# Layer two of a gated scan with two Strassen-like MLPs: who takes the finished sums out of PSUM

## The reference, cut to what matters

```python
# x, f_logit: (1, 6080, 256); lower_bound: (256); d_ff = 2048, fp32 throughout
f = lower_bound + (1 - lower_bound) * sigmoid(f_logit)
h[t] = f[t] * h[t-1] + (1 - f[t]) * x[t]            # a scan over 6080 tokens
# layer one: 6080 x 256 -> 2048 -> 256
a = h @ moe_w_in;  g = maximum(0.01 * a, a);  y = g @ moe_w_out
# layer two: the same shapes
a = y @ moe2_w_in
g = where(a >= 1, a, where(a <= -1, 0, (a + 1) ** 2 / 4))
out = g @ moe2_w_out                                # (6080, 256), row-major in HBM
```

## Time and profile before

| | |
|---|---|
| median of 3 runs | 1038.54 us |
| the profiled execution's own time | 1038.13 us |
| its span, first to last instruction | 1036.3 us |
| mean granted TensorE clock | 0.994 of full |
| TensorE matmul busy | 1004.5 us, 97% |
| VectorE busy | 802.8 us, 77% |
| ScalarE busy | 678.1 us, 65% |
| GpSimd busy | 197.5 us, 19% |

### The profile page before, as it was taken

How to read it: one execution, slowest core, us unless ns; L and a number is a source line. 1 busy time by engine, 2 the same in 40 slices (tenths; PEclk the granted TensorE clock), 3 DMA queues, 4 the chain that set the end, 5 groups by cost and what they waited for, 6 DMA issues and landing times.

```text
span 1036.3 us, 11820 instructions
## 1 busy us (share of the span) xinstructions
PE 1004.5 (97%) x4387; PEld 820.2 (79%) x4387; DVE 802.8 (77%) x823; ACT 678.1 (65%) x955; POOL 197.5 (19%) x191
## 2 busy tenths in 40 slices
PE   7999999999999999999989989999999999999996
PEld 6888788888888888888868868877877786887885
DVE  4766678678667677654688898898889889888885
ACT  5776777767767777756656665665666666666653
POOL 3404144333323300040040050040004005000000
PEclk8999999999999999999999999999999999999999
DMA  7433323334344230154330012011110201100112
GB/s 197 103 79 71 70 89 87 122 79 105 117 108 116 97 62 1 43 198 156 112 101 1 1 41 36 6 40 21 21 41 1 41 1 38 25 17 1 21 21 38
DMA packets 160605, 65.45 MB, mean 63 GB/s; under 512 B 142754, under 2 KB 150052, under 8 KB 160548
## 3 DMA queue, kind: packets, MB, share of 16 engines
q1 hardware_dynamic: 152516, 48.02, 19.5%
q0 software_dynamic: 3584, 15.73, 4.1%
q10 hardware_dynamic: 4448, 0.95, 0.5%
HBM read 40.70 MB, written 23.99 MB: 62 GB/s over the span
## 4 chain that ended last, share of the span: by engine, by line
PE 77%; DVE 12%; ACT 5%; issue 3%; DMA 1%; SPq 1%; POOL 0%; DVEq 0%; ACTq 0%
PE S L1074 39%; PE U L1058 34%; DVE G L863 3%; PE U L1025 3%; DVE H L858 2%; DVE H L838 2%; ACT G L592 2%; DVE extra L853 2%; ACT keep L557 2%; DVE H L846 1%; ACT extra L572 1%; DVE VF L820 1%; SPq L285 1%; DVE extra L878 1%; DMA extra<-in_f_logit_dram 1%
## 5 line engine op out<-in xcount | busy, mean ns | idle before, releaser
L1074 PE MATMUL S<-G,W_down 128*128 128x512 f32 (+2 forms) x2304 | 568.4, 388 | 3.3 <-DVE G L863 3.3
L1074 PEld LDWEIGHTS S<-G,W_down 128*128 128x128 f32 x2304 | 432.8, 188 | 92.4 <-DVE G L863 3.1
L1058 PE MATMUL U<-VF,W_up 128*128 128x512 f32 (+1 forms) x1848 | 467.1, 392 | 16.8 <-DVE H L846 10.0
L1058 PEld LDWEIGHTS U<-VF,W_up 128*128 128x128 f32 x1848 | 342.9, 188 | 103.4 <-ACT keep L557 14.1
L557 ACT ACTIVATE keep<-U 128x512 f32<-128x512 f32 (+1 forms) x352 | 207.6, 590 | 185.1 <-PE U L1058 184.8
L863 DVE TENSOR_TENSOR G<-H,G 128x1024 fp32r<-128x1024 f32 (+3 forms) x208 | 249.1, 1198 | 101.9 <-ACT G L592 100.7
L592 ACT ACTIVATE G<-H 128x1024 fp32r<-128x1024 f32 (+3 forms) x208 | 200.8, 985 | 7.4 <-DVE H L858 5.0
L572 ACT ACTIVATE extra<-extra,half 128x1024 f32<-128x1024 f32 (+1 forms) x96 | 109.3, 1140 | 118.2 <-DVE extra L853 117.9
L858 DVE SCALAR_TENSOR_TENSOR H<-H,extra 128x1024 f32<-128x1024 f32 (+1 forms) x96 | 123.1, 1291 | 34.5 <-ACT extra L572 34.5
L846 DVE TENSOR_TENSOR H<-U,keep 128x1024 f32<-128x1024 f32 (+1 forms) x88 | 107.2, 1218 | 44.9 <-ACT keep L557 43.8
L838 DVE TENSOR_TENSOR H<-U,keep 128x1024 f32<-128x1024 f32 (+1 forms) x88 | 106.7, 1213 | 29.4 <-PE U L1058 19.5
(11 more groups left out here) (76 smaller groups left out, 345.0 us busy)
## 6 DMA issues: line engine op xcount, KB each, us to landing
ready_up<-G POOLq DMA_DIRECT2D x8, 896.0 KB, 3.9
W_up<-ready_up SPq DMA_DIRECT2D x8, 896.0 KB, 5.0
extra<-in_f_logit_dram SPq DMA_DIRECT2D x44, 128.0 KB, 3.3
extra<-in_x_dram SPq DMA_DIRECT2D x44, 128.0 KB, 3.4
middle<-sent SPq DMA_DIRECT2D x22, 256.0 KB, 2.7
V<-middle SPq DMA_DIRECT2D x5, 1024.0 KB, 5.1
out_dram<-extra SPq DMA_DIRECT2D x40, 128.0 KB, 2.7
ready_down<-G POOLq DMA_DIRECT2D x8, 512.0 KB, 2.9
```

What stands on the lines that cost most here:

```text
L1058: mm = nc.tensor.matmul(U[:, bank, 0:w], w_form(j, wp, a), v_form(stage, vp, b), start=fresh and i == 0, stop=i == 2, skip_group_check=True)
L1074: mm = nc.tensor.matmul(S[:, 2 * d + h, 0:w], W_down[:, j, wp, at], g_of(u, e, gp)[:, h * w:(h + 1) * w], start=j == 0 and e == 0 and k == ...
```

## The change

For the stages of layer two but the last, `turn` now reads the finished bank in PSUM (`S`) instead of ScalarE's copy in `sent`, and ScalarE's four `take` calls in unit j = 1 are gone. The four turns of a stage move from the ends of units j = 2 and 3 into unit j = 1 of the next stage: two ahead of `add_second_chunk`, two behind it. TensorE, before it writes a bank anew, waits for the turn of that bank (`s_turned`) where it waited for the take (`s_taken`). Layer one, the first stage of layer two (which follows layer one's last tile) and the final turns are as they were. It concerns five places: the starts of the stages two to six of layer two.

```diff
 # ScalarE, unit loop of layer two
-                if u > SECOND + 1 and j == 1 and live:
-                    take(s - 1, 0)
-                    take(s - 1, 1)
...
-                if u > SECOND + 1 and j == 1 and live:
-                    take(s - 1, 2)
-                    take(s - 1, 3)
 # VectorE, turn()
-                if stage < STAGES - 1:
-                    dve.wait_ge(s_taken, tiles_before(stage) + i + 1)
-                    src = sent[:, 2 * d + h, 0:w]
-                else:
-                    dve.wait_ge(s_down, chunk_end(last_unit(stage), 1) - len(banks(stage)) + i + 1)
-                    src = S[:, 2 * d + h, 0:w]
+                dve.wait_ge(s_down, chunk_end(last_unit(stage), 1) - len(banks(stage)) + i + 1)
...
-                nc.vector.transpose(turned[:, at:at + w], src).then_inc(s_turned, 1)
+                nc.vector.transpose(turned[:, at:at + w], S[:, 2 * d + h, 0:w]).then_inc(s_turned, 1)
 # VectorE, unit loop of layer two
+                changed = live and s > STAGES1 and j == 1
+                if changed:
+                    turn(s - 1, 0)
+                    turn(s - 1, 1)
                 if live:
                     add_second_chunk(u)
+                if changed:
+                    turn(s - 1, 2)
+                    turn(s - 1, 3)
                 g_low(u - 1, 1)
...
-                if s > STAGES1 and j in (2, 3):
-                    turn(s - 1, 2 * (j - 2))
-                    turn(s - 1, 2 * (j - 2) + 1)
 # TensorE, down_banks()
-                            pe.wait_ge(s_taken, tiles_before(stage - 1) + prior.index((d, h)) + 1)
+                            at = prior.index((d, h)) + 1
+                            if stage - 1 < STAGES1:
+                                pe.wait_ge(s_taken, tiles_before(stage - 1) + at)
+                            else:
+                                pe.wait_ge(s_turned, tiles_before(stage - 1) - tiles_before(STAGES1) + at)
```

More of the change, by code:

```diff
@@ L599, in take @@
                     act.wait_ge(s_middle, 16 * tiles_before(stage))
-                elif stage > STAGES1:
-                    act.wait_ge(s_turned, tiles_before(stage) - tiles_before(STAGES1))
                 nc.scalar.activation(sent[:, 2 * d + h, 0:w], S[:, 2 * d + h, 0:w], ACT.Copy).then_inc(s_taken, 1)
```

## The result

The changed kernel takes 1043.18 us (median of 7 runs, 1040.46 to 1044.81) against 1039.98 us for the kernel before beside it (7 runs). The ratio is 1.0036 with a 95% interval of 1.0023 to 1.0049, so 3.7 us slower with 2.4 to 5.1 as interval. The forecast was 1042.4 us, 4.3 us slower, by the likeliest of its cases.

A forecast was written before the change was run, and what follows sets the result against it. TensorE was taken to set the time except where VectorE leads, in unit j = 1. Stages two to four 1.57, fifth 1.71 and last 1.03 us sum to 4.3: 1038.13 + 4.3 = 1042.4 us, range 1038.0 to 1046.5.

The forecast's parts named there:

- The turns in j = 1: Four turns on VectorE's path delay TensorE's j = 2 by 1.31 us (stages two to four), 2.44 (fifth), 1.40 (last).
- the pitch of a turn from PSUM: VectorE, start to start of 512-column turns: 0.64 us, bounds 0.61 and 0.74, or -0.6 and +2.0 us over 20 turns.
- The contention given back: Second `g_low` of j = 1, stages two to four, moves behind GpSimd's subtractions and takes 1.22 us instead of 2.19.
- rival B: GpSimd shuts out turns from PSUM, about 1 us lost in each of four stages: 1046.4 us; chance 0.10.
- The fifth stage: GpSimd ends before it matters; TensorE starts j = 2 by 2.44 us later, less 0.73 recovered: 1.71 us longer.
- The 0.7 to 0.8 us behind j = 2: TensorE's loss from j = 2 to the next j = 0, caused by paired turns, comes back: stretches about 61.5 us.
- Rival A: VectorE leads through the whole stage, so its own balance counts: 1037.3 us, no measurable change; chance 0.15.
- ScalarE's copies: Twenty copies in j = 1 go; they lay in ScalarE's waits, so removal is worth nothing on the path.
- rival D: Takes or stores mattered, say 1 us a stage of TensorE's waits: gain of about 2 us, 1036; chance 0.05.
- The earlier stores: All eight `store_out` transfers are issued about 20 us earlier; no engine waits for them soon: no cost.
- TensorE's new wait: Before chunk (u-1, 0), TensorE waits up to 1 us for banks 2 and 3, ahead of j = 2: no cost.
- C: Turns in j = 1 fall into an existing wait, lateness falls some 0.8 us a stage: 1038.4 us; chance 0.12.

The follow-up runs named there:

- run 5: Kernel before with GpSimd's last two subtractions of a stage cut from 512 to 8 columns: 1035.16 us, ratio 0.9961 to the kernel before.
- run 6: Changed kernel with GpSimd's last two subtractions of a stage cut from 512 to 8 columns: 1041.53 us, ratio 1.0021 to the kernel before.
- run 2: Changed kernel with four unused ScalarE copies per stage put back where the takes were: 1042.82 us, ratio 1.0032 to the kernel before.
- run 3: Kernel before, takes kept, with one turn at the end of each of units j = 2 to 5: 1035.71 us, ratio 0.9967.
- run 4: Kernel before, takes kept, with one turn behind the clips in each of units j = 2 to 5: 1034.8 us, ratio 0.9956.
- run 8: Changed kernel with turns 2 and 3 moved behind the second add: 1051.07 us, ratio 1.0107 to the kernel before.
- run 7: Changed kernel with each turn in j = 1 made twice, first into the unused tile `sent`: 1062.43 us, ratio 1.0222 to the kernel before.
- run 9: Kernel of run 4 with GpSimd's last two subtractions held until the products of units j = 2 and j = 4 finish: 1030.71 us, ratio 0.9912 to the kernel before.
- run 10: Kernel of run 4 measured again beside the kernel before: 1035.78 us, ratio 0.9962.
- run 1: Changed kernel measured once more without an edit: 1043.48 us, ratio 1.004 to the kernel before.

## Why the prediction was right

The mechanism and its places were right; the sum over the five stages was 0.8 us too high (4.3 forecast, 3.54 in the first profile, 3.4 in the second).

- *The turns in j = 1.* Forecast: TensorE's j = 2 later by 1.31 us in stages two to four, 2.44 in the fifth, 1.40 in the last. Measured, from each stage's first add: 1.16 in the third (1.14 and 1.17 in its neighbours), 2.19 in the fifth (882.37 - 863.29 against 877.43 - 860.54), 1.26 in the last (966.10 - 951.15 against 960.64 - 946.95). The term that was mis-sized is the pitch of a turn from PSUM: 0.64 in the sum, 0.61 measured, the lower bound of my range, four times a stage, which makes 0.6 us of the 0.8; the other 0.2 isn't traced to a row. The slope of 1 ns a column that I took from the adds does not hold for the turns, whose medians are 0.682 at 512 columns and 0.683 at 480. The Trainium skill (VectorE: DVE Perf Modes, the section on the TRN2 errata) gives VectorE 58 fixed cycles from SBUF and 120 from PSUM, by its 0.96 GHz an estimate of 65 ns more an instruction. That does not show in this operation at 512 columns: the trace differs by -6 ns.
- *The contention given back.* Forecast 0.97 us in three stages. Runs 5 and 6 show it: with GpSimd's subtractions cut, the kernel before gains 4.0 us in its stages (1.0 in each of stages two to five) and the changed one 1.1 (in the fifth alone), and their distance grows from 3.5 to 6.5 us by the profiles. The transposes from PSUM are not stretched where they run beside GpSimd (0.709 us at most), which refutes rival B.
- *The fifth stage.* Forecast 1.71 us longer, measured 1.45 and 1.34 in the two profiles of the changed kernel, but 0.35 in run 2. The forecast took GpSimd's work to lie as in the one profile of before and said that it comes to its end before it matters; the first `g_low` of j = 1 met it all the same and lasted 2.25 us. That both profiles of the changed kernel had the order of before is luck.
- *The 0.7 to 0.8 us behind j = 2.* They come back in full (61.52 and 61.55 us), and runs 3 and 4 get the same 61.53 from the kernel before. Rival A, in which VectorE leads through the stage, is refuted: by it stages two to four would each have become 0.4 us shorter, and they became 0.4 longer.
- *ScalarE's copies.* Their time is worth nothing (run 2): ScalarE's wait ahead of the square grows from 2.73 to 4.87 us. The copies of run 2 don't wait for the sums and nobody waits for them, so they don't test the other half of rival D, TensorE's waits for `take`. Against that half stands the profile of before, in which no idle time of TensorE's matmuls in these stages is ended by a take; its weight loads wait for one five times, 1.1 us in all. The earlier stores were tested by no run.
- *TensorE's new wait.* Up to 1 us forecast, 0.56 in the third stage; behind the group that it held up TensorE stands idle for 1.30 us more, until the add that it must wait for anyway. The forecast sign of 2.2 us idle ahead of j = 2 came out as 1.86, in two parts. Run 8 shows how thin the cover is.
- *C* assumed waits in j = 1 to fall into. There were none but the 0.16 us (0.30 and 0.18 in the last stage), and run 7 says the same of further turns.

The interval of the first comparison, 2.4 to 5.1 us, holds both the forecast 4.3 and the 3.5 of the profiles.

What stays open: that the fifth stage's 1 us in run 2 came from the order of those two starts is read from the timelines; no experiment moved GpSimd's start alone. That TensorE's lower clock accounts for the surplus of the slower executions of runs 7 and 8 over the profiled ones isn't shown. Nor is it shown where run 9 gained what its five stages don't hold.

## What to carry to other kernels

An engine with a low busy share over the whole kernel can lead in one unit of a stage and trail in all others; moving its work into that unit costs the whole pitch, while in the units where it trails the same work is free up to the slack (here 0.28 us a unit, and a 0.62 us hole behind the clips). Freeing an idle engine from copies brings nothing if the work goes to the one that is late. Look also for what the moved work pushes: here a stretched instruction fell out of GpSimd's way, and putting that right by itself gave about as much as the change cost: 3.2 us in the five stages between the profiles of runs 10 and 9 (5.1 by their medians), against 3.5.

## What the runs showed of the hardware that was not expected

TensorE's granted clock can fall to its lower level (0.50, 1.2 GHz) in the middle of a stage. In the fourth stage of run 7 it did so after gaps of 1.35, 0.33, 0.17, 1.37 and 0.24 us, and stayed at 0.50 from 797.60 to 803.38, with one more gap of 1.09 in it; behind 804.50 it was 1.00 again. In the third stage of run 8 it was at a mean of 0.58 over 3.5 us after one gap of 2.96. Like gaps need not bring it. The third stage of run 7 has the gaps of the fourth and the fourth stage of run 8 one of 3.02, both at 1.00 throughout. In the second stage of run 7 the clock fell after gaps of 1.38 and 0.33 alone, and two groups of six matmuls took 2.77 and 2.93 us instead of about 1.6, but TensorE had to wait for the turns there anyway and the stage lost nothing by it. In the profiled executions the falls cost 4.0 us in run 7 and 1.3 in run 8 beyond what the waits alone cost, and the runs are more scattered (1058 to 1066 us in run 7). In the last 21 us the same fall comes or doesn't and makes a difference of 1.6 us: behind a wait of 1.85 us, 24 matmuls take 5.49 us (run 1) or 7.04 (the first profile of the same kernel).

In the fifth stage, where VectorE's `g_low` with both sources in SBUF met GpSimd's sum, the one that had started first kept its 1.22 us and the other took longer: 2.12 us for `g_low` in run 1, 2.19 for GpSimd's sum in run 2. VectorE's adds and turns, which read PSUM, took 1.23 and 0.709 us at most in the changed kernel, beside GpSimd or not.
